# Attention, token mixer and gated net on one core: mixer and gated net put into one block, two value groups and x splits moved

## The reference

```
# token mixer
theta = x @ w_theta
y = einsum('ts,bsd->btd', w_tok_r, x * cos(theta)) + einsum('ts,bsd->btd', w_tok_i, x * sin(theta))
u = x + y
x2 = u + maximum(u @ w_ch, 0)
# gated net
h = maximum(x2 @ w_in, 0);  u, v = h[..., :512], h[..., 512:]
v_n = (v - mean(v)) / sqrt(var(v) + 1e-6)
gated = u * (w_spatial over time of v_n + b_spatial)
out = gated @ w_out
```

## Time and profile before

| what | us |
|---|---|
| median of 3 runs | 642.7 (642.45 to 643.78) |
| the profiled execution, its own time | 640.71 |
| its span | 639.0 |
| busy in it: PE / DVE / ACT | 594.3 / 367.5 / 290.2 |
| the mixer's first products (PE fillers) start | 122.09 |
| the gated net's first product starts | 386.07 |

### The profile page before, as it was taken

One profiled execution on the slowest core, in us unless ns is written; L12 is line 12 of the kernel. 1 busy time (PEld: TensorE's weight loads), 2 busy tenths in 40 slices (PEclk: granted clock), 3 DMA queues, 4 the chain that ended last, 5 costly groups with the idle time before them and its releaser, 6 DMA issues. The chain is left out here.

```text
span 639.0 us, 12023 instructions
## 1 busy us (share of the span) xinstructions
PE 594.3 (93%) x4262; PEld 571.2 (89%) x4262; DVE 367.5 (58%) x618; ACT 290.2 (45%) x513; POOL 35.8 (6%) x68
## 2 busy tenths in 40 slices
PE   1998999479989999999999989999999999999998
PEld 1888888379889999999999987998999899989998
DVE  7899997157769444844664354676425632562141
ACT  5799996345555333522542224633431343144112
POOL 2233332000000000000000000000000000000000
PEclk9999999779979999999999989999999999999999
DMA  7879987480321023023000514430021002000102
GB/s 191 203 221 253 252 243 236 134 263 0 92 95 38 25 75 95 34 70 95 16 21 30 173 63 132 138 115 0 2 82 68 0 0 74 0 0 14 63 0 75
DMA packets 32411, 58.77 MB, mean 92 GB/s; under 512 B 3824, under 2 KB 24304, under 8 KB 32368
## 3 DMA queue, kind: packets, MB, share of 16 engines
q1 hardware_dynamic: 32368, 58.21, 30.3%
HBM read 44.04 MB, written 14.16 MB: 91 GB/s over the span
## 5 line engine op out<-in xcount | busy, mean ns | idle before, releaser
L997 PE MATMUL mix_ps<-w_hi,z_hi 128*128 128x384 f32 x288 | 99.7, 346 | 2.5 <-DVE z_lo L77 2.5
L997 PE MATMUL mix_ps<-w_lo,z_hi 128*128 128x384 f32 x288 | 97.7, 339 | 0.0
L997 PE MATMUL mix_ps<-w_hi,z_lo 128*128 128x384 f32 x288 | 97.6, 339 | 0.0
L997 PE MATMUL gate_ps<-w_hi,w_lo 128*128 128x384 f32 x192 | 64.2, 334 | 0.0
L997 PE MATMUL gate_ps<-w_hi 128*128 128x384 f32 x192 | 64.1, 334 | 0.0
L997 PE MATMUL gate_ps<-w_lo,w_hi 128*128 128x384 f32 x192 | 64.1, 334 | 0.0
L997 PEld LDWEIGHTS mix_ps<-w_hi,z_hi 128*128 128x128 f32 x288 | 54.6, 190 | 3.7 <-issue 3.7
L997 PEld LDWEIGHTS mix_ps<-w_lo,z_hi 128*128 128x128 f32 x288 | 54.5, 189 | 0.0
L997 PEld LDWEIGHTS mix_ps<-w_hi,z_lo 128*128 128x128 f32 x288 | 54.4, 189 | 0.0
L72 ACT ACTIVATE g_hi<-gate 128x384 fp32r<-128x384 f32 x32 | 16.8, 526 | 76.1 <-DVE gate L1873 76.1
L1869 DVE TENSOR_TENSOR gate<-gate_ps,b_all 128x384 f32<-128x384 f32 x32 | 17.8, 556 | 56.9 <-PE gate_ps L997 56.5
(11 more groups left out here) (129 smaller groups left out, 1387.5 us busy)
## 6 DMA issues: line engine op xcount, KB each, us to landing
f_raw<-in_fT_dram SPq DMA_DIRECT2D x32, 144.0 KB, 3.7
k_raw<-in_kT_dram SPq DMA_DIRECT2D x32, 144.0 KB, 3.1
q_raw<-in_qT_dram SPq DMA_DIRECT2D x32, 144.0 KB, 3.6
v_raw<-in_vC_dram SPq DMA_DIRECT2D x16, 288.0 KB, 4.1
xT<-y_sb SPq DMA_DIRECT2D x32, 144.0 KB, 3.5
w_raw<-in_wB_dram SPq DMA_DIRECT2D x6, 768.0 KB, 6.5
xt<-xT SPq DMA_DIRECT2D x8, 576.0 KB, 4.1
u<-xT SPq DMA_DIRECT2D x8, 576.0 KB, 5.4
```

The lines of the kernel that those rows point to most:

```text
L997: done = pe.matmul(out, a, b, start=(first and n == 0), stop=(last and n == len(terms) - 1))
```

## The change

Six edits. (1) Mixer and gated net are programs of one block: the barrier between them, the mixer's wait for its last stores and the filler go away; the two banks theta_bank and small_ps are made outside and become the first two of the gated net's ring. Since buffers of the gated net lie where buffers of the mixer lay, waits take the barrier's place: SP waits for the last mix product before it loads wc_stage, PE for `add_channel` (x2_done) before it writes ring banks 2 and 3 and before the u groups, SP for the stores of x2T before it loads x2. (2) `first_values(0)` and `(1)`: value groups 0 and 1 of the gated net's batch 0 are made into these two banks, on PE between the last mix product and the channel products of the last batch. (3) `load_x2` one step sooner on SP, ahead of the stores of groups 3 to 5; `x2_up` and `x2_down` one step sooner on ACT and DVE. (4) `x_hi(0)` and `x_lo(0)` of the next batch move from behind group 5's sines and products to before weight part 4. (5) eps is set with the mixer's constants, the gated net's x counters are shared and opened in the mixer. (6) In the attention two semaphores become one with three thresholds; order and waits stay.

```diff
-def token_mix(nc, sems, waits_passed, w_hi, w_lo, w_raw, wb_hi, wb_lo, wB, wC, in_hi, in_lo, xt, xt_hi, xt_lo, xT, x2T):
+class Gates:
+
+
+
+    def __init__(self, nc, ctx, banks):
+        cnt = lambda name, per, ahead=2: Count(nc, ctx, "c_" + name, per, ahead)
+        self.banks = banks
+        self.xhi_done = cnt("xhi_done", 2)
+        self.xlo_done = cnt("xlo_done", 2)
+        self.v_ps = cnt("v_ps", ST)
+
+
+def v_group(pe, gates, xt_hi, xt_lo, in_hi, in_lo, bank, s):
+
+    def both(hi, lo, at, n):
+        return hi[:, at:at + n], lo[:, at:at + n]
+
+    three(pe, bank[:, :],
+          [(both(xt_hi, xt_lo, k * SEQ + s * 128, 128),
+            both(in_hi, in_lo, k * DFF + FH, FH)) for k in range(DT)]).then_inc(gates.v_ps.h, 1)
+
+
+def token_mix(nc, sems, block, gates, waits_passed, w_hi, w_lo, w_raw, wb_hi, wb_lo, wB, wC, in_hi, in_lo, xt, xt_hi, xt_lo,
+              half_pi, eps, xT, x2T):
...
+        theta_bank, small_ps = gates.banks
...
-        block = ctx.enter_context(nc.Block())
...
-            batches(sp, [(load(0), 0), (load_w_in(range(5)), 1)] + [(store(g), 2) for g in range(3)] + [(load(1), 0), (load_weights, 0)]
+            batches(sp, [(load(0), 0), (load_w_in(range(5)), 1)] + [(store(g), 2) for g in range(3)] + [(load(1), 0), (load_weights, 0), (load_x2, 1)]
                     + [(store(g), 2) for g in range(3, GROUPS)]
-                    + [(load_residual, 1), (load_w_in(range(5, W_IN_PARTS)), 1), (load_x2, 1)], 2)
-            for c in x2_out:
-                sp.wait_ge(c.h, c.per * (BATCH + 1))
+                    + [(load_residual, 1), (load_w_in(range(5, W_IN_PARTS)), 1)], 2)
+            sp.wait_ge(mix_done.h, mix_done.at(Step(None, 1, BATCH - 1), GROUPS))
...
-                        split_hi(act, half_of_tokens(xt_hi, th), half_of_tokens(xt, th)).then_inc(inhi_done, 1)
+                        split_hi(act, half_of_tokens(xt_hi, th), half_of_tokens(xt, th)).then_inc(gates.xhi_done.h, 1)
...
             batches(act, [
-                (weights_up(0), 0), (z_up(1), 1), (to_turns(2), 1), (u_up(0), 2), (u_up(1), 2), (x2_up, 2), (trigs(2), 1), (xn_out(3), 1), (weights_up(2), 1),
+                (weights_up(0), 0), (z_up(1), 1), (to_turns(2), 1), (u_up(0), 2), (u_up(1), 2), (trigs(2), 1), (xn_out(3), 1), (weights_up(2), 1),
                 (z_up(2), 1), (to_turns(3), 1), (trigs(3), 1), (xn_out(4), 1), (weights_up(3), 1), (w_in_up(0), 1), (w_in_up(1), 1),
-                (z_up(3), 1), (to_turns(4), 1), (trigs(4), 1), (xn_out(5), 1), (weights_up(4), 1), (w_in_up(2), 1), (w_in_up(3), 1),
-                (z_up(4), 1), (to_turns(5), 1), (trigs(5), 1), (x_hi(0), 0), (xn_out(0), 0), (weights_up(5), 1), (w_in_up(4), 1),
+                (z_up(3), 1), (to_turns(4), 1), (trigs(4), 1), (xn_out(5), 1), (x_hi(0), 0), (weights_up(4), 1), (w_in_up(2), 1), (w_in_up(3), 1),
+                (z_up(4), 1), (to_turns(5), 1), (trigs(5), 1), (xn_out(0), 0), (weights_up(5), 1), (w_in_up(4), 1),
                 (z_up(5), 1), (to_turns(0), 0), (trigs(0), 0), (xn_out(1), 0), (w_in_up(5), 1), (w_in_up(6), 1), (w_in_up(7), 1),
-                (z_up(0), 0), (to_turns(1), 0), (trigs(1), 0), (xn_out(2), 0), (x_hi(1), 0), (weights_up(1), 0), (weights_up(6), 1)], 2)
+                (z_up(0), 0), (to_turns(1), 0), (trigs(1), 0), (xn_out(2), 0), (x_hi(1), 0), (x2_up, 1), (weights_up(1), 0), (weights_up(6), 1)], 2)
 
         @block.tensor
         def _(pe):
-            for c in (turn_ps, theta_ps, mix_used, mix_done, ch_ps):
...
+            def first_values(s):
+                def f(b):
+                    if last_batch(b):
+                        for c in (gates.xhi_done, gates.xlo_done):
+                            pe.wait_ge(c.h, c.at(Step(None, 1, 0), 1))
+                        if s == 0:
+                            pe.wait_ge(r1_done.h, r1_done.at(b, ST))
+                            pe.wait_ge(inhi_done, W_IN_PARTS)
+                            pe.wait_ge(inlo_done, W_IN_PARTS)
+                        else:
+                            pe.wait_ge(xn_done.h, xn_done.at(b, ST))
+                            pe.wait_ge(x2_done.h, x2_done.at(b.back(1), GROUPS))
+                        v_group(pe, gates, xt_hi, xt_lo, in_hi, in_lo, gates.banks[s], s)
+                return f
...
             batches(pe, [
                 (mix(0, 0), 1), (theta(2), 1), (mix(0, 1), 1), (turn(3), 1), (mix(0, 2), 1),
-                (mix(1, 0), 1), (theta(3), 1), (channel(0), 2), (mix(1, 1), 1), (turn(4), 1), (mix(1, 2), 1), (channel(1), 2),
+                (mix(1, 0), 1), (theta(3), 1), (first_values(0), 2), (first_values(1), 2), (channel(0), 2), (mix(1, 1), 1), (turn(4), 1), (mix(1, 2), 1), (channel(1), 2),
                 (mix(2, 0), 1), (theta(4), 1), (channel(2), 2), (mix(2, 1), 1), (turn(5), 1), (mix(2, 2), 1), (channel(3), 2),
                 (mix(3, 0), 1), (theta(5), 1), (channel(4), 2), (mix(3, 1), 1), (turn(0), 0), (mix(3, 2), 1), (channel(5), 2),
                 (mix(4, 0), 1), (theta(0), 0), (mix(4, 1), 1), (turn(1), 0), (mix(4, 2), 1),
                 (mix(5, 0), 1), (theta(1), 0), (mix(5, 1), 1), (turn(2), 0), (mix(5, 2), 1)], 2)
-            pe.wait_ge(r1_done.h, r1_done.at(Step(None, 1, BATCH - 1), ST))
-            keep_warm(pe, theta_bank, w_hi, 16)
...
                     for th in range(2):
-                        dve.wait_ge(inhi_done, W_IN_PARTS + th + 1)
+                        dve.wait_ge(gates.xhi_done.h, gates.xhi_done.at(Step(None, 1, 0), th + 1))
                         split_lo(dve, half_of_tokens(xt_lo, th), half_of_tokens(xt, th), half_of_tokens(xt_hi, th))\
-                            .then_inc(inlo_done, 1)
+                            .then_inc(gates.xlo_done.h, 1)
...
             batches(dve, [
-                (weights_down(0), 0), (z_down(1), 1), (reduce(2), 1), (u_down(0), 2), (u_down(1), 2), (x2_down, 2), (multiply(2), 1), (weights_down(2), 1),
+                (weights_down(0), 0), (z_down(1), 1), (reduce(2), 1), (u_down(0), 2), (u_down(1), 2), (multiply(2), 1), (weights_down(2), 1),
                 (z_down(2), 1), (reduce(3), 1), (add_channel(0), 2), (multiply(3), 1), (add_channel(1), 2),
                 (weights_down(3), 1), (w_in_down(0), 1), (w_in_down(1), 1),
-                (z_down(3), 1), (reduce(4), 1), (add_channel(2), 2), (multiply(4), 1), (add_channel(3), 2),
+                (z_down(3), 1), (reduce(4), 1), (add_channel(2), 2), (multiply(4), 1), (add_channel(3), 2), (x_lo(0), 0),
                 (weights_down(4), 1), (w_in_down(2), 1), (w_in_down(3), 1),
-                (z_down(4), 1), (reduce(5), 1), (add_channel(4), 2), (multiply(5), 1), (x_lo(0), 0), (add_channel(5), 2), (weights_down(5), 1), (w_in_down(4), 1),
+                (z_down(4), 1), (reduce(5), 1), (add_channel(4), 2), (multiply(5), 1), (add_channel(5), 2), (weights_down(5), 1), (w_in_down(4), 1),
                 (z_down(5), 1), (reduce(0), 0), (multiply(0), 0), (w_in_down(5), 1), (w_in_down(6), 1), (w_in_down(7), 1),
-                (z_down(0), 0), (reduce(1), 0), (add_mix(0), 1), (add_mix(1), 1), (multiply(1), 0), (add_mix(2), 1),
+                (z_down(0), 0), (reduce(1), 0), (x2_down, 1), (add_mix(0), 1), (add_mix(1), 1), (multiply(1), 0), (add_mix(2), 1),
                 (add_mix(3), 1), (x_lo(1), 0), (weights_down(1), 0), (add_mix(4), 1), (add_mix(5), 1), (weights_down(6), 1)], 2)
 
...
+        return x2_done, x2_out
...
-        ring = ps("ringc", 4)
+        ring = gates.banks + ps("ringc", 2)
...
             sp.dma_start(b_all[:, :], bass.AP(bias.tensor, 0, [[0, 128], [1, SEQ]])).then_inc(b_in, 16)
+            for c in x2_out:
+                sp.wait_ge(c.h, c.per * (BATCH + 1))
             batches(sp, [(load_next, 0), (store, 2)], 2)
...
             def v_in_ring(b):
-                for s in range(ST):
+                for s in range(len(gates.banks) if first(b) else 0, ST):
...
-                    three(pe, ring[s % 4][:, :],
-                          [(both(xt_hi, xt_lo, k * SEQ + s * 128, 128),
-                            both(in_hi, in_lo, k * DFF + FH, FH)) for k in range(DT)]).then_inc(v_ps.h, 1)
+                    if s < 4 and first(b):
+                        pe.wait_ge(x2_done.h, x2_done.at(Step(None, 1, BATCH - 1), s - 1))
+                    v_group(pe, gates, xt_hi, xt_lo, in_hi, in_lo, ring[s % 4], s)
 
             def u_in_ring(b):
+                if first(b):
+                    pe.wait_ge(x2_done.h, x2_done.at(Step(None, 1, BATCH - 1), GROUPS))
...
-        token_mix(nc, sems, waits_passed, w_hi, w_lo, w_raw, wb_hi, wb_lo, wB, wC, in_hi, in_lo, xt, xt_hi, xt_lo, x_by_batch, x2T)
-        gated_net(nc, sems, waits_passed, w_hi, w_lo, in_hi, in_lo, xt, xt_hi, xt_lo, wC, bias, x2T, out)
+        half_pi = sems.enter_context(nc.sbuf_tensor("half_pi", [128, 1], F32))
+        eps = sems.enter_context(nc.sbuf_tensor("eps", [128, 1], F32))
```

(6 more changed lines are left out.)

53 lines of the change are left out of this document (21 added, 32 removed).

## The result

| | before | changed |
|---|---|---|
| median, us | 642.58 | 635.17 (633.49 to 638.08, 4 runs) |
| ratio, 95% interval | | 0.9888 (0.9845 to 0.9930) |
| the profiled execution, its span, us | 640.71, 639.0 | 638.08, 636.3 |

The account below looks back on a forecast made before the run. PE was taken to bound the gated net from 386 us, with its idle time in the mixer and at the handover. Handover -6.5 and mixer +0.1 gave -6.4, from 642.7 to 636.3 us; 8-in-10 range 634.0 to 639.2.

Parts of the forecast that it names:

- Handover, -6.5: Mixer to gated net: without barrier and filler, with two value groups moved ahead, second statistics and what follows come 6.5 us sooner.
- PE would have allowed 8.1: Handover: on PE alone, the four other value groups start at 382.15 instead of 390.25, a gain of 8.1 us.
- the opening: Handover: ACT's first copy of values waits until DVE opens the fourth counter, between 382.8 and 383.3; 383.0 taken.
- the statistics ring: Gated net's start: DVE and ACT wait for each other from the second statistics on; all moved by 6.5 us.
- The 1.6 us that I called lost to the clock at the handover: Handover before: behind PE's 2.08 us stop, 17 products took 4.55 us at a lowered clock, 1.6 us lost.
- Mixer, +0.1: Token mixer: splitting x sooner puts PE 5.5 us ahead, but a later stop gives it back; net 0.1 us more.
- the stop of theta: Mixer: PE's 3.56 us stop before batch 1's first theta goes; one of some 4.0 us comes near 190.
- The stop of 0.33 us at a mix product: Mixer, mix product of 172.50: comes 1.05 us later, so PE's stop of 0.33 us becomes 1.4.
- The clock at the stop ahead of u's fifth group: Rival, gated net: the clock falls at PE's new stop of about 1.9 us, costing 1.6 to 2.8 us; chance 0.20.
- The weight part behind the store: Rival, handover: first weight part starts only when the store lands, 1.1 us after ACT wants it, total 637.4; chance 0.08.
- A kept mixer gain: Rival, mixer: with more DVE slack between 181 and 212, PE's 5.5 us would stand, total 630.7; chance 0.10.
- Slower by the clock: Rival: clock falls at new stops, up to 2.8 us each; from three uncovered falls on the kernel is slower; chance 0.03.

Follow-up runs that it names:

- the second run: The changed kernel itself measured once more, with nothing altered: 636.07 us, ratio 0.9896 to before.
- e1: Changed kernel with x_hi(0) and x_lo(0) back at their old places, behind group 5's sines and products: 635.15 us, ratio 0.9897 to before.
- e5: Changed kernel with the last x2 copy's lower half and first two mix sums on DVE ahead of the next batch's first z_lo: 634.59 us, ratio 0.9912.
- e12: Changed kernel with only the last part of w_in split later, behind the next batch's z of the first block: 632.23 us, ratio 0.9853 to before.
- e3: Changed kernel with the two value groups moved behind the channel products on PE: 636.14 us, ratio 0.9904 to before.
- e4: Changed kernel with the gated net's eight DVE counters opened at the mixer's start: 636.32 us, ratio 0.9912 to before.
- e2: Kernel before with only x_hi(0) and x_lo(0) moved sooner: 642.79 us, ratio 1.0009 to before.
- e6: Changed kernel with copies, statistics, normalising and splits of value groups 0 and 1 among the last channel additions: 637.77 us, ratio 0.9942 to before.
- e11: Changed kernel with statistics and first three weight parts among the channel additions, and w_in's last part split behind the next z: 630.78 us, ratio 0.9821.

## Why the prediction was right, point by point

Times behind the last mix product (368.43 in the forecast's account, 372.21 in the trace):

| step | forecast | measured |
|---|---|---|
| first channel product | 4.35 | 4.31 |
| value group 2 | 13.72 | 13.85 |
| last channel addition | 13.93 | 14.04 |
| first copy of values | 14.57 | 14.48 |
| second statistics | 16.17 | 16.08 |
| first weight part lands | 18.7 | 19.4 |
| u's fifth group | 30.4 | 30.64 |
| spatial products, by the chain | 37.0 | 37.16 |

- **Handover, -6.5:** measured -6.3, from the distances. The mechanism held: PE would have allowed 8.1, and DVE's last addition, the opening and the statistics ring took 1.8 of it back. Two terms were off. The weight part was issued 0.85 us behind the last store, not at once, so it had nothing to spare but made ACT wait 0.28 us. This reached nobody: u's fifth group stands 30.63 to 30.64 us behind the last mix product with a wait of 0.28 us, of 0.17 (the second run) and of none (e1, e5, e12), and DVE's fourth statistics follow the third by 3.33 us, as before. The missing 0.2 lies in the ring, which I had moved as a whole: from the second statistics to u's fifth group it takes 14.56 us, before 14.24. DVE's reciprocal for the fourth group starts 0.39 us behind the aggregate, before 0.10, and the profile shows nothing that it waited for (timeline of DVE):

```profile
394.89 0.18 DVE L1856 BATCH_NORM_AGGREGATE mean_var<-stats 128x2 f32<-128x6 f32 x1 [0.17 <-DVE stats L1850]
395.28 0.16 DVE L1864 RECIPROCAL rstd<-std 128x1 f32<-128x1 f32 x1 [0.21 <-issue]
```

  The same 0.38 to 0.39 us stand there in e1, e3, e4, e5 and e12; why stays open. A slip without effect: DVE opens eight counters for the gated net now, not nine, and vn_done is the fourth of these eight; in the kernel before it was the fifth of nine. The 1.6 us that I called lost to the clock at the handover were not on the path in the kernel before, as e2 shows; the sum does not use them.
- **Mixer, +0.1:** the stop of theta went, one of 3.66 us came (forecast 4.0), 18 slow products cost 2.8 us as in the row it was taken from. The stop of 0.33 us at a mix product became 0.86 and 1.11 (forecast 1.4). Fill products to turn(4) are 0.9 us more in one run and 1.0 less in the other, which is mostly the start-up: from theta of batch 1's first half it is 36.52 and 36.23. e1 and e2 show no worth by time. Right, and the small number can't be told from nothing.
- **The clock at the stop ahead of u's fifth group** (0.20): not in six executions with a stop of 1.81 to 1.84 us there (both of the changed kernel, e1, e5, e6, e12), but in e4 with 1.85. So it came in one of seven, about what I gave it; whether chance or the length of the stop decides here, seven executions can't tell.
- **The weight part behind the store:** the store was issued at 386.84 and landed 1.9 us later, at 388.7. A part that starts only then would land at 392.6; it landed at 391.6, 3.9 us after its own issue (3.8 before). I had taken the rule of ring order (the Trainium skill, DMA: Bandwidth & Descriptors, Queues, rings and completion order) to speak for a delay. The same sentence goes on that data descriptors carry no barrier, so that a later one may finish before an earlier one; so it does not say that a part waits for the store to land, and the trace, with 0.1 us, shows no such wait.
- **A kept mixer gain** fell because DVE and ACT had no slack, as argued from the stop of 0.67 us. But I had read only who waited and not what began it. The same group of rows held the load wait of 2.84 us on ACT, and e12 shows that moving this wait behind z_hi was worth 3.4 to 3.7 us (2.0 in e11, where the clock fell behind turn(4)).
- **Slower by the clock:** behind the start-up, each execution of the changed kernel had one stop with slow products, and no execution of another kernel had more than two (the kernel before, e1, e2, and e4 with its falls at the mix product and ahead of u's fifth group). It would have taken three.
